# Windowed attention and two feed-forward layers on one core: a reordered head with pair-by-pair loads

## The reference

```python
keep = (pos[None, :] < n_sink) | ((rel >= 0) & (rel < window))   # rel = row - column
a = softmax(where(keep, q @ k.T / 8, -1e9))
x = (a @ v) as 1536 x 512
x = (silu(x @ w_gate) * (x @ w_val)) @ w_out
h = x @ w_in2
out = (maximum(h, 0) + alpha * minimum(h, 0)) @ w_out2
```

## Time and profile before

| | us |
|---|---|
| median of 3 runs | 630.95 (630.51 to 631.57) |
| profiled execution, its own time | 630.74 |
| its span | 629.0 |
| PE busy in the span | 619.4 |
| DVE busy | 408.2 |
| POOL busy | 452.6 |
| ACT busy | 244.6 |

### The profile page before, as it was taken

The page is one execution under the profiler, slowest core; times in us unless marked ns, Lnnn a source line. Parts: engine busy times, 40 slices in busy tenths (PEclk is TensorE's granted clock), DMA queues, the critical chain, the costliest instruction groups (busy, mean ns, idle before and its releaser), DMA issues.

```text
span 629.0 us, 9375 instructions
## 1 busy us (share of the span) xinstructions
PE 619.4 (98%) x3066; PEld 486.9 (77%) x3066; DVE 408.2 (65%) x693; ACT 244.6 (39%) x589; POOL 452.6 (72%) x600
## 2 busy tenths in 40 slices
PE   8899999999999999999999999999999999999997
PEld 5567777777777888888887888887888888888886
DVE  5845656657485957464747474898687567756474
ACT  5644654545535532121303030445544424442150
POOL 6967788877688989998989583799999987810000
PEclk9999999999999999999999999999999999999999
DMA  9073432311323112121202331100222222000004
GB/s 307 23 236 118 135 126 81 131 36 52 83 68 84 34 35 83 51 68 34 68 33 68 100 88 48 50 2 17 68 67 68 69 67 86 16 1 0 2 17 184
DMA packets 29007, 45.67 MB, mean 73 GB/s; under 512 B 2880, under 2 KB 8768, under 8 KB 28960
## 3 DMA queue, kind: packets, MB, share of 16 engines
q1 hardware_dynamic: 28672, 44.81, 22.8%
q10 hardware_dynamic: 288, 0.26, 0.1%
HBM read 41.92 MB, written 3.15 MB: 72 GB/s over the span
## 4 chain that ended last, share of the span: by engine, by line
PE 94%; DVE 3%; ACT 2%; issue 1%; DVEq 0%; ACTq 0%
PE ffn_ps L2029 29%; PE att_ps L2004 24%; PE ffn_ps L1944 15%; PE att_ps L2029 8%; PE ffn_ps L2004 6%; PE att_ps L1889 3%; PE att_ps L1850 3%; PE att_ps L1865 2%; PE att_ps L1944 1%; PE att_ps L1899 1%; ACT scratch L2073 1%; PE att_ps L2036 1%; DVE top L2260 1%; PE att_ps L1844 0%; DVE scratch L2276 0%
## 5 line engine op out<-in xcount | busy, mean ns | idle before, releaser
L1708 POOL TENSOR_TENSOR w_lo<-raw_weights,w_hi 128x512 fp32r<-128x512 f32 (+1 forms) x128 | 155.5, 1215 | 10.3
L1707 POOL CAST w_hi<-raw_weights 128x512 fp32r<-128x512 f32 (+1 forms) x128 | 79.9, 624 | 29.3 <-PE ffn_ps L2029 17.2
L2394 DVE TENSOR_TENSOR scratch<-ffn_ps,scratch 128x512 f32<-128x512 f32 x108 | 74.0, 687 | 34.7 <-PE ffn_ps L2029 34.1
L1736 POOL TENSOR_TENSOR w_lo<-part_sum,w_hi 128x256 fp32r<-128x256 f32 x80 | 59.7, 747 | 6.4
L1944 PE MATMUL ffn_ps<-x_hi,w_hi 128*128 128x512 f32 x152 | 61.7, 406 | 0.8 <-ACT x_hi L2098 0.7
L1944 PE MATMUL ffn_ps<-x_hi,w_lo 128*128 128x512 f32 x152 | 59.5, 391 | 0.0
L1944 PE MATMUL ffn_ps<-x_lo,w_hi 128*128 128x512 f32 x152 | 58.7, 389 | 0.0
L2029 PE MATMUL ffn_ps<-h_hi,w_hi 128*128 128x512 f32 x130 | 51.6, 397 | 0.0
L1788 POOL TENSOR_TENSOR scratch<-scratch,inv 128x264 f32<-128x264 f32 (+1 forms) x48 | 29.9, 624 | 30.0 <-DVE inv L2265 29.8
L2029 PE MATMUL ffn_ps<-h_hi,w_lo 128*128 128x512 f32 x130 | 50.7, 390 | 0.0
L2029 PE MATMUL ffn_ps<-h_lo,w_hi 128*128 128x512 f32 x130 | 50.6, 389 | 0.0
(11 more groups left out here) (208 smaller groups left out, 1573.3 us busy)
## 6 DMA issues: line engine op xcount, KB each, us to landing
raw_weights<-pieces SPq DMA_DIRECT2D x122, 256.0 KB, 2.7
k_sb<-kt SPq DMA_DIRECT2D x12, 264.0 KB, 3.2
out<-scratch SPq DMA_DIRECT2D x12, 256.0 KB, 2.1
q_sb<-qt SPq DMA_DIRECT2D x11, 256.0 KB, 3.5
v_sb<-vt SPq DMA_DIRECT2D x10, 256.0 KB, 4.0
v_sb<-vt SPq DMA_DIRECT2D x1, 512.0 KB, 4.6
scratch<-vs SPq DMA_DIRECT2D x1, 384.0 KB, 6.2
q_sb<-qt ACTq DMA_DIRECT2D x2, 128.0 KB, 2.9
```

The costliest lines, as they stand in the source:

```text
L1707: chain(pool.tensor_copy(hi, raw[:, r % n_raw, at]))
L1708: last = pool.tensor_tensor(lo, raw[:, r % n_raw, at], hi.bitcast(F32), ALU.subtract)
L1736: pool.tensor_tensor(lo, s, hi.bitcast(F32), ALU.subtract).then_inc(split_done, 1)
L2394: ins = dve.tensor_tensor(to, back_ps(key), total, ALU.add)
```

## The change

The first load of keys and queries is cut in three steps instead of two: pair 0, pair 1, pairs 2 and 3. The zero products go from 6, 6 and 4 to 4, 4 and 1. The sink products of a quad stand one slot later (behind slots 8, 12, 16), and `round_x` and `rest_of_x` of that quad move with them (`rest_of_x` to behind slots 9, 13 and, as before, 18). On DVE, `low_sinks` stands at the end of its slot, behind inversion and spread, instead of ahead of them. The scores of unit 16 stand behind the values of unit 15. In the head POOL splits 3 weight pieces instead of 6 (slots 1, 2, 5, 6, 16, 17); slots 20, 22 and 24 get two jobs instead of one, so that the number of jobs done is the same from slot 24 on.

```diff
--- before.py
+++ after.py
@@ -964,16 +964,20 @@
 
 
 
-    last_head = early + HEAD_LAG - 1
-    late_rest = []
-    for w in range(last_head):
-        rest = emit_slot(head_slot(w))
-        if late_rest and (late_rest[0][1] < quads_t - 2 or w == last_head - 1):
-            plan.extend(late_rest)
-            late_rest = []
-        late_rest += rest
+    n_head = early + HEAD_LAG
+    low_after = {}
+    for w in range(n_head):
+        plan.append(head_slot(w))
+        done = w - HEAD_LAG
+        for c in range(quads_t):
+            if tile(c) > 0 and done == scores_until(c):
+                plan += [("sinks", c), ("x", c)]
+                low_after[n_head - 2 if c == quads_t - 2 else w + 1] = ("x_rest", c)
+        if w in low_after:
+            plan.append(low_after[w])
+    plan.append(("x", quads_t - 1))
     emit_slot(slot(early, early, n_units))
-    plan.extend(emit_slot(head_slot(last_head)))
+    plan.append(("x_rest", quads_t - 1))
 
 
     part_one = []
@@ -1288,6 +1292,10 @@
 
 
     first_pieces = parts["B"] * F
+
+    head_pieces = first_pieces - 3
+    half_slots = (1, 2, 5, 6, early, early + 1)
+    sink_slots = (3, 4, early + 2, early + 3)
     plan_at = {}
     for n, (what, key) in enumerate(plan):
         if what in ("front", "back", "strip"):
@@ -1300,9 +1308,9 @@
         name = ("piece", key) if what == "piece" else ("sums", (key[0], key[1], key[2] // 2))
         return plan_at[cell_ahead[name]] if name in cell_ahead else -1
 
-    next_job = first_pieces
-    for n in range(early + HEAD_LAG, len(slot_plan)):
-        for _ in range(1 if n % 2 == 0 or plan[slot_plan[n] + 1][0] == "tsum" else 2):
+    next_job = head_pieces
+    for n in range(n_head, len(slot_plan)):
+        for _ in range(1 if n > n_head + 4 and n % 2 == 0 or plan[slot_plan[n] + 1][0] == "tsum" else 2):
             if next_job < len(jobs) and ready_at(jobs[next_job]) < slot_plan[n]:
                 in_slot[n].append(jobs[next_job])
                 next_job += 1
@@ -1482,8 +1490,7 @@
                 return (gate_sb if kind_of((g, part)) == "G" else value_sb)[:, V_TILE, :]
             return strip_ps((g, part), ROLE[f, t])
 
-        first_in = sem("first_pairs_in")
-        others_in = sem("other_pairs_in")
+        step_in = [sem(f"first_quad_in{n}") for n in range(3)]
         first_v_in = sem("first_values_in")
         k_in = [sem(f"k_in{r}") for r in range(RING)]
         q_in = [sem(f"q_in{r}") for r in range(RING)]
@@ -1534,7 +1541,7 @@
         block = ctx.enter_context(nc.Block())
 
 
-        first_pairs, other_pairs = slice(0, n_pairs // 2), slice(n_pairs // 2, n_pairs)
+        steps = (slice(0, 1), slice(1, 2), slice(2, n_pairs))
 
         def loads_until(c):
 
@@ -1614,9 +1621,8 @@
                 sp.dma_start(raw[:, r % n_raw, :], pieces[piece_of[raws[r][:3]]]).then_inc(raw_in[r % n_raw], 16)
 
 
-            for pairs in first_pairs, other_pairs:
-                sp.dma_start(k_sb[:, pairs, 0:2, :], kt[0, :, pairs, :, :]).then_inc(
-                    first_in if pairs == first_pairs else others_in, 16)
+            for n, pairs in enumerate(steps):
+                sp.dma_start(k_sb[:, pairs, 0:2, :], kt[0, :, pairs, :, :]).then_inc(step_in[n], 16)
             sp.dma_start(v_sb[:, 0:2, :, :], vt[0:2].rearrange("t p a n -> p t a n")).then_inc(first_v_in, 16)
             load_piece(0)
             load_keys(1)
@@ -1797,7 +1803,6 @@
                     pool.tensor_copy(p_sink[:, c % 2, :].rearrange("p (r a n) -> p r a n", r=3, n=n_sink),
                                      sinks.unsqueeze(1).to_broadcast([P, 3, 2 * n_pairs, n_sink])).then_inc(gathered, 1)
 
-            halves_split, sinks_split = 0, 0
             n_slot = -1
             for what, units in plan:
                 if what == "tsum":
@@ -1807,16 +1812,14 @@
                 n_slot += 1
                 if units[1] is not None:
                     normalise(units[1])
-                if n_slot < early + HEAD_LAG:
-                    if n_slot in (3, 4, early + 2, early + 3):
-                        split_v_sink(sinks_split // 2, sinks_split % 2)
-                        sinks_split += 1
-                    elif halves_split < 2 * first_pieces and n_slot not in (0, 13, 14, 15):
-                        split_piece(jobs[halves_split // 2][1], 2, halves_split % 2)
-                        halves_split += 1
-                else:
-                    for job in in_slot[n_slot]:
-                        do(job)
+                if n_slot in sink_slots:
+                    n = sink_slots.index(n_slot)
+                    split_v_sink(n // 2, n % 2)
+                if n_slot in half_slots:
+                    n = half_slots.index(n_slot)
+                    split_piece(jobs[n // 2][1], 2, n % 2)
+                for job in in_slot[n_slot]:
+                    do(job)
             for job in late_jobs:
                 do(job)
 
@@ -1825,8 +1828,8 @@
             def scores(u):
                 c, g = divmod(u, n_pairs)
                 r = place(c)
-                if c == 0 and g in (0, n_pairs // 2):
-                    pe.wait_ge(first_in if g == 0 else others_in, 32)
+                if c == 0 and g < len(steps):
+                    pe.wait_ge(step_in[g], 32)
                 elif g == 0:
                     if loads_until(c):
                         pe.wait_ge(k_in[r], 16 * loads_until(c))
@@ -1850,7 +1853,7 @@
                         last = pe.matmul(ps[:, 0:2 * P + n_sink], q, both[:, n_sink:], start=True, stop=True)
                     last.then_inc(scores_done[h], 1)
 
-            fills = {2: 6, 3: 4}
+            fills = {2: 4, 3: 1}
 
             def turn(u):
                 c, g = divmod(u, n_pairs)
@@ -1890,15 +1893,17 @@
                                          start=g == 0 and m == 0, stop=not has_prev(c), skip_group_check=True)
                         if m == len(halves_of) - 1:
                             last.then_inc(pv_done[h], 1)
-                if g == n_pairs - 1:
-                    if has_prev(c):
-                        if tile(c) == 1:
-                            pe.wait_ge(vsink_split, 2 * (c // n_tiles + 1))
-                        pe.wait_ge(sink_done, sinks_until(c))
-                        for a in range(n_pairs):
-                            last = pe.matmul(x[:, a, :], v_sink[:, c // n_tiles, block_cols(a)], pts[:, c % 2, :], start=False,
-                                             stop=True, skip_group_check=True)
-                        last.then_inc(x_done, 1)
+                if g == n_pairs - 1 and has_prev(c) and c >= quads_t:
+                    sink_values(c)
+
+            def sink_values(c):
+                if tile(c) == 1:
+                    pe.wait_ge(vsink_split, 2 * (c // n_tiles + 1))
+                pe.wait_ge(sink_done, sinks_until(c))
+                for a in range(n_pairs):
+                    last = pe.matmul(x_ps(c)[:, a, :], v_sink[:, c // n_tiles, block_cols(a)], pts[:, c % 2, :],
+                                     start=False, stop=True, skip_group_check=True)
+                last.then_inc(x_done, 1)
 
             PASSES = ((0, 0), (0, 1), (1, 0))
 
@@ -2036,7 +2041,7 @@
                     pe.matmul(ps, h_hi[:, 0, 0:P], h_hi[:, 0, :], start=True, stop=True, skip_group_check=True)
 
             pe.wait_ge(zeros_done, 1)
-            keep_busy(6, bank(att_ps, 2))
+            keep_busy(4, bank(att_ps, 2))
             for what, n in plan:
                 if what == "front":
                     front(*n)
@@ -2044,6 +2049,8 @@
                     back(*n)
                 elif what == "strip":
                     strip(*n)
+                elif what == "sinks":
+                    sink_values(n)
                 elif what == "slot":
                     if n[0] in fills:
                         keep_busy(fills[n[0]], bank(att_ps, 2))
@@ -2198,19 +2205,15 @@
                         act.wait_ge(tlo_done, thi_no[stage, "T3", kk])
                 act.activation(operands[name][0][:, kk, :], sum_sb(stage, n)[:, kk, :], ACT.Copy).then_inc(thi_done, 1)
 
-            for pairs in first_pairs, other_pairs:
-                act.dma_start(q_sb[:, place(0), pairs, :], qt[tile(0), :, pairs, :]).then_inc(
-                    first_in if pairs == first_pairs else others_in, 16)
+            for n, pairs in enumerate(steps):
+                act.dma_start(q_sb[:, place(0), pairs, :], qt[tile(0), :, pairs, :]).then_inc(step_in[n], 16)
             for what, n in plan:
-                if what == "slot" and n[0] is not None and n[0] != early:
+                if what == "slot" and n[0] is not None:
                     if sinks_in_slot(n[0]) is not None:
                         high_sinks(sinks_in_slot(n[0]))
                     exps(n[0])
                 elif what == "x":
                     round_x(n)
-                    if n == quads_t - 1:
-
-                        exps(early)
                 elif what == "x_rest" and n >= quads_t:
```

(4 more changed lines are left out.)

## The result

The changed kernel took 634.96 us (median of 17 executions, 631.28 to 637.39), the kernel before beside it 630.72 (17 executions, 630.18 to 633.42): a ratio of 1.006, 95% interval 1.0043 to 1.0077. It is slower, and outside the range of 629.2 to 631.9.

What follows compares the result with a forecast made beforehand. DVE was taken to pace the head (22 to 34 us), PE everything behind 38.3 us; -0.3 - 0.1 + 0 + 0.6 - 0.45 = -0.25 on the profiled 630.74, with 0.21 for the median, gave 630.7 us; range 629.2 to 631.9.

Steps and rivals of the forecast that it cites:

- the loads: Entry: three steps let scores(0) start earlier, partly offset by slower early products; net -0.3 us (0 to -0.55).
- the clock behind PE's waits: Head: PE's waits counted only as lengths, hidden or given back; a lower clock was considered only from the entry.
- the longer SP queue: Entry: one more issue of 0.49 us ahead of values, weights and next keys costs nothing, at most 0.49.
- The landing: Entry: 196 KB less ahead of scores(0) lands 0.55 us earlier (bounds nothing and 0.57).
- Fewer zero products: Entry: fewer ahead of the first scores mostly hidden; DVE has unit 3 behind it earlier, -0.1 us (0 to -0.3).
- Slots 8 to 14: Later sinks move PE's stall to the transposes, 0.5 to 0.7 us long; net 0 (-0.3 to +0.3).
- Third sinks: End of head: turn(13) +0.1 us, at 34.4; turn(14) and all that follows +0.6 (+0.3 to +0.9).
- scores(16): End of head: behind values(15) they fall into the wait for round_x; -0.45 us (-0.2 to -0.66).
- Weights: POOL: fewer pieces in the head, two jobs in slot 20 fit its idle time; cost 0, or a late piece's lateness.
- Rival (2): From scores(4) on, about 10.3 us, PE stays at 1.2 GHz from the start; 632.7 us, chance 0.09.

Runs made afterwards that it cites:

- b_fills: The kernel before with only the zero products cut from 6, 6 and 4 to 4, 4 and 1; 631.53 us, ratio 0.9998.
- b_loads: The kernel before with only the first load in three steps instead of two; 631.73 us, ratio 1.0013.
- b_jobs: The kernel before with only the weight pieces shared out as in the change; 630.97 us, ratio 0.9995.
- c_both: The changed kernel with zero products put into its waits: 8 ahead of scores(4), 2 ahead of values(11), 4 ahead of turn(13); 631.69 us, ratio 1.0007.
- The fourth group: Four kernels with zero products put into PE's waits and the order kept, three from the changed kernel; entry and late waits filled together: 631.69 us.
- a_low: The changed kernel with only low_sinks put back ahead of inversion and spread; 633.92 us, ratio 1.0048.
- both_low: The changed kernel with the old loads, the old zero products and low_sinks back ahead of inversion and spread; 631.02 us, ratio 1.0004.
- c_entry: The changed kernel with 8 zero products put into the wait ahead of scores(4) only; 635.17 us.
- b_sinks: The kernel before with only the sinks a slot later and low_sinks last in its slot; 631.83 us, ratio 1.0023.
- a_again: The changed kernel, unchanged, timed and profiled once more against the kernel before; 634.11 us, ratio 1.0043.
- a_both: The changed kernel with the old zero products (6, 6, 4) and the old two-step load; 633.08 us, ratio 1.0024.
- a_fills: The changed kernel with the old zero products (6, 6, 4), three-step load kept; 632.48 us, ratio 1.0022.

## Why the prediction was wrong

Two things failed: a step that decided the result, the clock behind PE's waits, and a term that was mis-sized, the loads. The terms come first.

**The loads: a term of the wrong size and sign.** I put the three steps at -0.3 and the longer SP queue at nothing. The landing itself came as forecast: with four zero products ahead of them, scores(0) start at 3.52 with three steps and at 4.14 with two (b_fills, behind a wait of 0.55 for the keys), 0.62 for my 0.55. But I had read scores(0) of the kernel before as standing behind the loads. They had landed at 0.80 + 3.2 = 4.0, and PE was in the six zero products until 4.45; so scores(0) came at 3.52 and not at 3.8 to 3.9, and in b_loads, with its six zero products, not earlier at all. They took 1.24 instead of 0.99. And I priced a DMA by its bytes at the rate of the earlier trace rows, and looked for those queued behind only as far as the first values. The rate itself fell, 381 to 170 GB/s between 3.00 and 4.40, and the keys and queries of the next quad, which scores(4) need, landed later. Their rows, with KB and us from issue to landing, in the kernel before (issued at 2.84 and 3.54):

```profile
k_sb<-kt SPq DMA_DIRECT2D x1, 264.0 KB, 5.2
q_sb<-qt SPq DMA_DIRECT2D x1, 256.0 KB, 5.3
```

and in the changed kernel, issued at 3.20 and 3.90:

```profile
k_sb<-kt SPq DMA_DIRECT2D x1, 264.0 KB, 6.8
q_sb<-qt SPq DMA_DIRECT2D x1, 256.0 KB, 7.4
```

The wait ahead of scores(4), 0.28 before, became 2.04. This pair of profiles overstates the difference: over the ten profiles with two steps these queries took 5.3 to 8.4 us, 6.8 on average, and over the eight with three 7.0 to 8.0, 7.5 on average. They land 1.0 us later on average, and single profiles overlap. By itself (b_loads) the edit costs +0.76, on the other side of both its bounds (0 to -0.55). How that divides is open: in its profile scores(4) wait only 0.21 for the queries, and the six zero products ahead of scores(2) take 2.24 instead of 1.66, a longer time at the lower level.

**Fewer zero products: swallowed.** scores(4) of b_fills start at 11.23, not earlier than the 10.88 of before, and the time without products turned into waiting (1.09 ahead of them). -0.1 forecast, 0 to +0.6 measured.

**Slots 8 to 14: right in place.** The stall stands ahead of the transposes and none ahead of the sink products; it is 0.31 and 0.83 long, either side of the 0.5 to 0.7. **Third sinks: right in sign and about in size.** turn(13) at 34.49 for 34.4, turn(14) 0.7 later than before for 0.6; the edit alone costs +0.83 without a fall (631.72 against 630.89). **scores(16): right**, -0.46 for -0.45. **Weights: right but for one wait**: PE stands 0.47 for POOL at 62.49, behind a piece that POOL took up at 57.34 after waiting 2.72 for its DMA; by itself (b_jobs) it can't be told from nothing.

The costs of the parts alone (+0.76, +0.83, -0.46, +0.08) sum to +1.21, with the zero products left out, whose size is open; the changed kernel without a fall is 0.8 slower than before (631.48 against 630.72), and c_both 0.7. That they overlap, a slot that waits at one place waiting less at the next, is likely but not shown. With every size right, the forecast would thus have been about 631.5: inside the range, and "same". So it is not the loads that put the measurement outside.

**The clock: the step that failed.** The other 3.5 us (634.96 against 631.48) are the falls. Rival (2) named the mechanism and gave 632.7 at a chance of 0.09, but looked for it only at the entry, as a low level that would last on from the start. The rest of the text treated each wait as a length of time that is either hidden or not: 0.5 to 0.7 us "hidden" or "given back". What it cost was something else. Behind waits of 0.6 to 2.5 us on PE, hidden or not, 7 to 17 us of this head ran at 1.2 GHz in some executions. The kernel before has waits too, the longer of them 0.42 to 0.66 us, and fell 7 times in 129; in the change the longest are 0.8 to 2.5, and it fell 22 times in 27. The length of one wait doesn't decide it alone: b_fills has one of 1.09 at the entry and no fall in 12.

The Trainium skill, "TensorE: Matmul & The Clock Gate", section "What's actually happening", has it that idling brings the throttle back. By that rule the edit of the sinks, not only that of the entry, speaks against the change. The fourth group agrees: 22 of 27 with the waits, 0 of 13 with products in them. I quoted the rule and applied it to one place.

What stays open: why one execution of a kernel falls and the next doesn't; what the entry adds, since a_low (5 of 6) falls where both_low (1 of 12) doesn't, at late waits of equal length, while c_entry, with its entry filled, falls as often as the changed kernel; and why the three-step load lowers the rate with the DMA engines still busy.

## What to carry to other kernels

Before PE's order is changed, list PE's waits by length in both versions, not only the sum and not only those on the path: here waits that grew from 0.5 to 1 us ahead of an unbroken row of products cost 3 to 4 us behind them in 5 of 12 executions (b_sinks, 635.0 to 635.8 against 631.7), at 1.2 GHz. Read the spread and the mean granted clock of many executions: one profile of such a kernel shows either case. If an order with such a wait is wanted for another reason, put products without use into it; here 14 of them gave back 2.4 to 3.3 us. And a first load in smaller steps brought the first step earlier and what stood behind it later: ask first what else holds the engine at the start, and follow the transfers until the queue is empty.

## What the runs showed that I had not expected

- A fall is a matter of chance: 8 of 10, 10 of 12, 5 of 12, 4 of 12, 1 of 12, 0 of 13 for kernels that differ in a few waits, with single times of one kernel from 630.23 to 638.62.
- The clock doesn't fall at the wait but behind it: 1.6 us after its end in a_again, with PE busy in between; it stays at 0.50 for about 7 us (a_again) to 17 (c_entry), worked out from the clock of the stages, although PE is busy nearly all of that time.
- a_both, whose long waits are 0.84 at the second sinks and 0.57 and 0.98 within 2.2 us at the third, fell in 8 of 12. One execution of c_entry fell at 30.8, behind a wait of 0.84 and before the third sinks; c_both has the same 0.84 and no fall in 13.
- How long PE stays at the lower level from the start varies between executions: scores(0) at 4.38 take 0.71 in a_fills, the upper level already, while c_entry was at the lower until about 10 and c_both until about 13.
- Between 3.00 and 4.40 the DMA engines move 145 to 215 GB/s in the eight profiles with three steps and 372 to 385 in the ten with two, while their busy share is 0.85 to 0.95 against 1.05 to 1.13.
